# Where SyncE issues the second block's loads: before or behind the engines' meeting

## The reference

```
attention   state[b,h] = w * state + k_t v_t^T ;  y_t = r_t (state + (u k_t) v_t^T)      4 batches, 8 heads of 48
experts     where x.w_skip > 0: e = argmax(x W_gate), x += p_e * relu(x W1[e]) W2[e]      8 experts, 384 -> 1024 -> 384
gated       a = x w1 ; b = x w2 ; out = ((a * b) w3) w_out                                384 -> 1024 -> 1024 -> 384
```

## Time and profile before

| | us |
|---|---|
| median of 3 runs | 617.03 (615.47 to 617.14) |
| profiled execution | 613.97 |
| its span, first to last instruction | 612.2 |
| mean granted TensorE clock | 0.992 |

### The profile page before, as it was taken

One profiled execution on the slowest core, in us unless ns is written; L12 is line 12 of the kernel. 1 busy time (PEld: TensorE's weight loads), 2 busy tenths in 40 slices (PEclk: granted clock), 3 DMA queues, 4 the chain that ended last, 5 costly groups with the idle time before them and its releaser, 6 DMA issues. The chain is left out here.

```text
span 612.2 us, 17257 instructions
## 1 busy us (share of the span) xinstructions
PE 590.4 (96%) x7295; PEld 526.9 (86%) x7295; DVE 294.7 (48%) x474; ACT 227.0 (37%) x410; POOL 156.4 (26%) x179
## 2 busy tenths in 40 slices
PE   6699999999999999999699999999999999999997
PEld 5699999766999999999388888888888888888886
DVE  5478889283777777774033323323323323232212
ACT  3155666444665555552052222121312212222212
POOL 6568887215055444441050000000000000000000
PEclk9899999999999999999899999999999999999999
DMA  7779997596566777740530013004004001001001
GB/s 130 133 143 187 186 184 190 209 315 233 175 242 251 279 273 269 234 137 20 113 51 1 1 55 49 0 2 103 1 1 103 1 0 52 1 0 51 2 1 52
DMA packets 133218, 67.80 MB, mean 111 GB/s; under 512 B 111228, under 2 KB 127232, under 8 KB 133176
## 3 DMA queue, kind: packets, MB, share of 16 engines
q1 hardware_dynamic: 105320, 57.91, 33.0%
q10 hardware_dynamic: 25552, 4.72, 4.1%
q0 software_dynamic: 2304, 4.59, 2.3%
HBM read 55.92 MB, written 12.20 MB: 111 GB/s over the span
## 5 line engine op out<-in xcount | busy, mean ns | idle before, releaser
L1613 DVE TENSOR_TENSOR gl_g_sb<-gl_a_sb,gl_pab 128x512 f32<-128x512 f32 x48 | 33.0, 688 | 173.9 <-ACT gl_a_sb L1575 173.9
L1524 PE MATMUL gl_pab<-gl_xT_hi,wm_lo 128*128 128x512 f32 x288 | 113.0, 392 | 0.0
L1524 PE MATMUL gl_pab<-gl_xT_lo,wm_hi 128*128 128x512 f32 x288 | 112.9, 392 | 0.0
L1524 PE MATMUL gl_pab<-gl_xT_hi,wm_hi 128*128 128x512 f32 x288 | 112.1, 389 | 0.0
L1575 ACT ACTIVATE gl_a_sb<-gl_pab 128x512 f32<-128x512 f32 x48 | 28.8, 599 | 186.0 <-PE gl_pab L1524 186.0
L1524 PEld LDWEIGHTS gl_pab<-gl_xT_hi,wm_lo 128*128 128x128 f32 x288 | 54.0, 188 | 11.4
L1524 PEld LDWEIGHTS gl_pab<-gl_xT_hi,wm_hi 128*128 128x128 f32 x288 | 54.1, 188 | 10.5 <-DVE gl_xT_lo L1620 0.3
L1524 PEld LDWEIGHTS gl_pab<-gl_xT_lo,wm_hi 128*128 128x128 f32 x288 | 54.0, 188 | 10.4
L1278 PE MATMUL ex_ph<-ex_xT_hi,ew_w_hi 128*128 128x224 f32 x192 | 52.9, 275 | 0.0
L1278 PE MATMUL ex_ph<-ex_xT_hi,ew_w_lo 128*128 128x224 f32 x192 | 52.7, 274 | 0.0
L1278 PE MATMUL ex_ph<-ex_xT_lo,ew_w_hi 128*128 128x224 f32 x192 | 52.7, 274 | 0.0
(11 more groups left out here) (200 smaller groups left out, 1232.5 us busy)
## 6 DMA issues: line engine op xcount, KB each, us to landing
w_in<-in_moe_w SPq DMA_DIRECT2D x8, 1536.0 KB
ew_w_in<-in_moe_w SPq DMA_DIRECT2D x8, 1536.0 KB
w_in<-in_moe_w SPq DMA_DIRECT2D x14, 512.0 KB, 9.1
k_in<-in_k SPq DMA_DIRECT2D x48, 96.0 KB, 3.3
v_in<-in_v ACTq DMA_DIRECT2D x48, 96.0 KB
r_in<-in_r SPq DMA_DIRECT2D x48, 96.0 KB, 3.1
out<-gl_o_sb SPq DMA_DIRECT2D x12, 384.0 KB, 2.5
w_in<-xbuf SPq DMA_DIRECT2D x60, 64.0 KB, 2.4
```

The source lines that it names most:

```text
L1524: m = pe.matmul(p_ab[f % 2][w][:, :], a[:, w * KD + k, cols], b[t.slot][:, k, :], start=(k == 0 and n == 0), stop=(k == KD - 1 and n == 2))
L1613: dve.tensor_tensor(g_sb[f % 2][:, :], a_sb[f % 2][:, :], p_ab[f % 2][1][:, :], ALU.mult).then_inc(s_g, 1)
```

## The change

The twelve loads of block 1 are no longer issued at the end of SyncE's first-block program. SyncE's gated program no longer skips block 1: its `load` call, the first thing that this program does, issues the same twelve DMAs. Block 0's two loads stay where they were. No wait is added: for block 1 the count is 3 - 6, and `wait` does nothing.

```diff
@@ experts(), end of SyncE's program
             for s in s_out:
                 sp.wait_ge(s, 32 * env["n_scattered"])
             env["gated_x"].load_first(sp, xbuf)
-            env["gated_x"].load(sp, xbuf, 1, 1)
@@ gated_layers(), SyncE's program
                 def load(t):
-                    if isinstance(t.c, int) and t.num() < 2:
+                    if isinstance(t.c, int) and t.num() == 0:
                         return
                     if isinstance(t.c, int) and t.num() == 2:
                         sp.wait_ge(s_T, 2)
```

## The result

| | kernel before | changed kernel |
|---|---|---|
| first comparison, median | 616.93 us (615.47 to 617.14, 4 runs) | 608.86 us (608.56 to 608.94, 4 runs) |
| second comparison, median | 616.08 us (614.07 to 618.10, 17 runs) | 609.07 us (608.21 to 609.57, 6 runs) |
| profiled execution of the first | 613.97 us, span 612.2 | 608.56 us, span 606.8 |

The ratio is 0.9873 (95% interval 0.9856 to 0.9890) in the first comparison and 0.9882 (0.9860 to 0.9905) in the second: faster by 1.2 to 1.3%, 7 to 8 us. The forecast was 611.0 us with a range of 609.3 to 613.2, so the direction was right and the gain came out too small; 608.86 lies under the range. The two profiled executions differ by 5.41 us only. The gap between 5.4 and 7 to 8 us is the question of this study.

A forecast was written before the change was run, and what follows sets the result against it. PE was taken as the bound, full except for a 4.75 us hole at the first block's end. Gains of 4.38 + 1.61 = 5.99 us, say 6.0, off the 617.03 us median gave 611.0 us, range 609.3 to 613.2.

The forecast's parts named there:

- Removed issues, PE next to set the meeting: First block's end: without twelve issues SyncE signals at about 296.2, PE last at 298.7, its next matmul at 298.97.
- Term one: PE's idle time at the meeting falls from 4.75 to 0.37 us: gain 4.38 us, bounds 4.2 to 4.5.
- other-side rival: Block 1's loads land too late for VectorE's first transpose, stopping the engines; 618.7 us at 2.2 times, chance 0.03.
- Term two, the clock: Four matmul records behind the meeting run at full clock, 1.29 instead of 2.90 us: gain 1.61, bounds 0 to 1.9.
- What is late next: Behind the meeting: block 0's loads land by 299.3, PE wants them at 300.3, margin 1.0 us; then ScalarE's split of x.
- Taking a fixed stretch off the median: Whole kernel: the 6.0 us shift is fixed, so it comes off the median of 617.03 us, giving 611.0 us.
- Added and moved work: Behind the meeting: twelve issues and later loads cost zero; packets beside PE's work cost zero, bounds −0.1 to +0.2 us.
- A: Behind the meeting, code is not at hand for ScalarE, VectorE or SyncE; about 612.5 us, chance 0.10.
- B: PE's clock falls anyway behind the new gap, so only the idle time is gained; 612.6 us, chance 0.04.
- C: The meeting ends on another engine, as GpSimd's arrival is not shown; nothing gained, 617.0 us, chance 0.03.
- D: Block 1's loads miss VectorE's first transpose, then ScalarE and PE stop; 618.7 us at 2.2 times, chance 0.03.

The follow-up runs named there:

- tiny12: Changed kernel plus twelve DMAs of 16 rows of 64 bytes on SyncE where block 1's loads used to stand; 613.8 us, ratio to before 0.9966.
- ahead8: Changed kernel with eight of block 1's twelve loads issued ahead of the meeting, four behind; 613.91 us, ratio 0.9957.
- ahead4: Changed kernel with four of block 1's twelve loads issued ahead of the meeting, eight behind; 609.69 us, ratio 0.9894.
- again: Kernel before, no edit, profiled a second time; 615.93 us.
- again2: Kernel before, no edit, profiled a third time; 616.15 us.
- again3: Kernel before, no edit, profiled a fourth time; 616.92 us.
- swap: Kernel before with block 1's twelve loads issued first, then block 0's two, all ahead of the meeting; 615.83 us (one run).
- warm: Kernel before with 38 extra transposes on PE behind its last matmuls of the first block; 613.81 us, ratio 0.9967.
- both_behind: Changed kernel with block 0's two loads also moved behind the meeting, to the head of SyncE's gated program; 613.7 us, ratio 0.9956.

## Why the prediction was wrong in size

**Removed issues, PE next to set the meeting: right.** Forecast restart 298.97, measured 299.00; gap 0.37, measured 0.41 in all three traces of the changed kernel. SyncE signalled at 296.8, not 296.2, since the second of block 0's issues took 1.19 us instead of 0.50; it had no effect. `tiny12`, `ahead8` and `ahead4` confirm that the issues ahead of the meeting are the cause.

**Term one, 4.38 us (bounds 4.2 to 4.5): mis-sized.** It took the length of the hole from one execution. The row itself carried the warning: an issue of 989 ns against a median of 488, which I used for the other-side rival only. In three more traces that issue took 1.25 to 2.21 us. The mean hole of the four is 5.61 us; less 0.41 the term is 5.2 us.

**Term two, the clock, 1.61 us (upper bound 1.9): right in mechanism, mis-sized.** The low clock lasted 3.4 us in the trace read and 6.8 in `again`, `again2`, `again3`, `ahead8` and `swap`. From restart to gates the four traces of before need 6.41 us in the mean, the three of the changed kernel 4.24: 2.2 us. The claim that the transposes gain nothing was true of the first trace alone; they take 2.1 to 2.6 us in the others. There is an error the other way too: I priced the first four records at 1.29 us, the pace of four that follow other matmuls without a pause, and behind an idle time they took 1.53 us at full clock in all three traces of the changed kernel. In the first pair of traces the records give 1.37 us, not 1.61.

**What is late next: the margin of 1.0 us on block 0's landing was wrong.** I took the landing of 3.0 to 3.8 us from one pair of loads. In the changed kernel's traces the slower of the pair took 5.7, 4.5 and 4.3 us. In the first of them the chain ran through it, and from restart to gates PE needed 4.47 us instead of 4.13: 0.34 us. This and the 0.24 us of the first four records are why the gates stood at 303.47 instead of the forecast 302.9, and the profiled pair shows 5.4 us and not 6.0.

**Taking a fixed stretch off the median: this is the step that failed.** I saw that the median lay 3.06 us above the profiled execution and treated that surplus as independent of the change. Much of it was the change's own subject, a longer hole and a longer low clock, and went with it: the mean stretch of the four traces of before is 12.03 us, against 10.30 in the one that I read, so 1.7 of the 3.06 us. Another 1.2 us is in the median of three runs itself, 617.03 where 32 later runs gave 615.83. Whether that is chance or the device is not shown. With means over the traces the two terms are 5.2 + 2.2 = 7.4 us, against 7.0 us in the second comparison; in the three traces of the changed kernel the first block happens to end 0.6 us later in the mean than in the four of before. The 8.07 us of the first comparison are these 7.0 and the 1.1 us by which its four runs of before (616.93) lay above the later 32.

**Added and moved work: right.** The twelve issues behind the meeting cost nothing, the next twelve follow at once, the 36 gate matmuls take 8.19 us beside the loads, and VectorE's transpose stands at 314.33 without a wait.

**The rivals.** A (code not at hand) did not come: ScalarE began 1.42 us behind the first transpose in the first trace of the changed kernel, later than the 1.16 before by the wait for the load, and 1.08 and 1.07 us behind it in the two traces without that wait. SyncE's first issue of line 1096 stood at 299.0, at once behind its release at 298.9. By the rule of the Trainium skill (Runtime: NRT & Kernel Launch, Instruction fetch mechanics) a stall was possible behind a taken branch to code outside the fetched window; no row here shows one at this meeting. The price that I took for it, PE's branch of 3.46 us, is one of PE's program and not of its matmuls: PE was busy for all of the 8.60 us from 290.00 to 298.60 around it. B did not come: the clock stayed at 1.00 in the three traces of the changed kernel and in `ahead4`. C and D did not come.

## What to carry to other kernels

Ahead of a meeting of the engines, leave in each program only what must be there; a DMA issue was an instruction of about half a microsecond in its engine's program here, now and then of one to two, and the others waited for the issue, not for the data. Leave ahead as many as fit before the last engine arrives, and first those whose data is wanted at once. When the median of the runs lies well above the profiled execution, the trace may show a lucky case: ask which idle time or low clock varies between executions before a fixed number is taken off, and widen the range upwards in gain if the change removes it.

## What the runs showed of the hardware that I had not expected

- SyncE's issue of a small DMA mostly took 0.42 to 0.49 us. Where small loads followed two loads of 384 KB at once, one issue took 0.99 to 2.21 us in all eight traces: the fifth in six (four of before, `warm`, `ahead8`), the fourth in `ahead4`, the first in `both_behind`. With the small ones first (`swap`) the second took 0.96 us; with tiny ones (`tiny12`) none was slow.
- The slower of the two loads of 384 KB landed 3.7 to 6.0 us after issue over the thirteen traces. In the eight above the slow issue goes with it: 3.8, 3.7, 4.9, 5.0, 5.6, 5.2, 5.7 and 6.0 us of landing for slow issues of 0.99, 1.01, 1.25, 1.42, 1.59, 1.70, 2.02 and 2.21 us. Which causes which, or what causes both, is not shown.
- Idle times of PE of 0.41 us (three traces), 0.42 us and 1.49 us left the granted clock at 1.00. With 3.6 us or more it fell to 0.5, for 3.4 us in two traces and 6.8 us in five, and not by the length of the hole: 3.4 us with holes of 3.60 and 4.75, 6.8 us with 3.77 and 4.59. In `both_behind` it fell behind two waits of 2.10 and 1.18 us with four transposes between.
